# A different split of the first expert's weights, a shorter choice of that expert and larger, earlier clears in an attention and mixture-of-experts kernel

## What is computed

```python
h = x @ w_in                      # 512 x 2048
P = a[0] + a[1] * h + a[2] * h2 + a[3] * h3
Q = 1.0 + np.abs(b[0]) * np.abs(h) + np.abs(b[1]) * h2
g = P / (Q + 1e-06)
return (g @ w_out)                # 2048 x 512
```

## Time and profile before

| | us |
|---|---|
| three runs | 1037.04, 1037.2, 1035.95 (median 1037.04) |
| the profiled execution's own time | 1036.77 |
| its span in the profile | 1035.1 |
| PE busy in the span | 1003.8 (97%) |
| DVE, ACT, POOL busy | 647.5, 583.5, 410.9 |

### The profile page before, as it was taken

How to read it: one execution, slowest core, us unless ns; L and a number is a source line. 1 busy time by engine, 2 the same in 40 slices (tenths; PEclk the granted TensorE clock), 3 DMA queues, 4 the chain that set the end, 5 groups by cost and what they waited for, 6 DMA issues and landing times.

```text
span 1035.1 us, 19854 instructions
## 1 busy us (share of the span) xinstructions
PE 1003.8 (97%) x6222; PEld 819.4 (79%) x6223; DVE 647.5 (63%) x1207; ACT 583.5 (56%) x1255; POOL 410.9 (40%) x397
## 2 busy tenths in 40 slices
PE   8988999999999999999999999997999999999998
PEld 5777778888888888888888778786888888888886
DVE  5876788878867877887688679855223424325221
ACT  7877778766676667667666667624223324225221
POOL 3676444444543454455345357722111111112111
PEclk9999999999999999999999999998999999999999
DMA  8999614700920290064009942117311512411111
GB/s 301 357 403 348 256 41 135 232 1 11 314 84 0 100 307 0 10 234 163 0 18 373 366 149 72 41 42 294 123 41 48 190 42 84 159 41 40 31 48 37
DMA packets 58528, 143.26 MB, mean 138 GB/s; under 512 B 4967, under 2 KB 10727, under 8 KB 58480
## 3 DMA queue, kind: packets, MB, share of 16 engines
q1 hardware_dynamic: 51680, 121.07, 33.0%
q0 software_dynamic: 6800, 21.56, 6.2%
HBM read 71.08 MB, written 72.32 MB: 139 GB/s over the span
## 4 chain that ended last, share of the span: by engine, by line
PE 76%; issue 7%; SPq 5%; ACT 4%; DMA 3%; DVE 3%; POOL 1%; ACTq 0%; DVEq 0%; POOLq 0%
PE PS L511 20%; PE PS L670 19%; PE PS L542 14%; PE PS L551 13%; SPq L463 4%; PE PS L535 2%; ACT prob L819 2%; PE PS L613 2%; PE PS L690 2%; DMA x_raw<-w_exp 1%; PE PS L528 1%; DVE PS L1001 1%; DMA qk<-qk_all 1%; PE PS L583 1%; DMA e_raw<-w_exp 1%
## 5 line engine op out<-in xcount | busy, mean ns | idle before, releaser
L511 PE MATMUL PS<-xs,weights 128*128 (+1 forms) x1152 | 282.7, 394 | 0.0
L511 PEld LDWEIGHTS PS<-xs,weights 128*128 128x128 f32 x1152 | 212.6, 188 | 43.1
L670 PE MATMUL PS<-weights,g_hi 128*128 128x512 f32 x768 | 238.6, 392 | 7.6 <-POOL g_lo L1344 4.6
L1344 POOL TENSOR_TENSOR g_lo<-g_sb,g_hi 128x512 fp32r<-128x512 f32 x96 | 123.9, 1291 | 272.8 <-ACT g_hi L899 272.8
L670 PEld LDWEIGHTS PS<-weights,g_hi 128*128 128x128 f32 x768 | 142.8, 188 | 43.2 <-POOL g_lo L1344 9.1
L670 PE MATMUL PS<-weights,g_lo 128*128 128x512 f32 x384 | 149.6, 390 | 0.0
L542 PE MATMUL PS<-weights,xg_hi 128*128 (+1 forms) x448 | 143.3, 401 | 0.5 <-issue 0.2
L880 ACT ACTIVATE b_ln<-PS,cf 128x512 f32<-128x512 f32 x96 | 65.9, 686 | 132.8 <-PE PS L511 132.8
L551 PE MATMUL PS<-weights,h_hi 128*128 (+1 forms) x432 | 136.1, 396 | 0.1
L1347 POOL TENSOR_TENSOR den<-den,b_r 128x512 f32<-128x512 f32 x96 | 127.7, 1330 | 2.1 <-ACT b_r L907 2.1
L1099 DVE SCALAR_TENSOR_TENSOR den<-den,b_r 128x512 f32<-128x512 f32 x96 | 70.2, 731 | 50.9 <-POOL den L1347 50.9
(11 more groups left out here) (190 smaller groups left out, 1605.0 us busy)
## 6 DMA issues: line engine op xcount, KB each, us to landing
rows_by_expert<-pad_rows SPq DMA_DIRECT2D x40, 1028.0 KB, 15.1
e_raw<-w_exp SPq DMA_DIRECT2D x34, 512.0 KB, 6.7
qk<-qk_all SPq DMA_DIRECT2D x32, 480.0 KB, 6.6
vw<-v_all SPq DMA_DIRECT2D x32, 384.0 KB, 6.0
rows_by_expert<-pad_rows SPq DMA_DIRECT2D x8, 1285.0 KB, 18.2
w_raw<-w_mlp SPq DMA_DIRECT2D x16, 512.0 KB, 8.4
pad_rows<-rows_by_expert POOLq DMA_DIRECT2D x30, 257.0 KB
x_raw<-attention_out_t SPq DMA_DIRECT2D x10, 512.0 KB, 4.5
```

The source lines that it names most:

```text
L511: last = pe.matmul(PS[:, H_BANK + f % 2, :], w[:, wp], rhs, start=k == 0, stop=k == 3 * KT - 1)
L670: last = pe.matmul(PS[:, ACC_BANK + s, :], gp[:, f % 2, s * P:(s + 1) * P], w[:, wp], start=f == 0 and k == 0, stop=f == FT - 1 and k == 2)
L1344: pool.tensor_tensor(g_lo[:, q], g_sb[:], g_hi[:, q].bitcast(F32), ALU.subtract).then_inc(g_lo_done, 1)
```

## The change

```diff
-E_ACT = {4: 0, 6: 1, 8: 2, 9: 3, 10: 4, 12: 5, 13: 6, 14: 7}
-E_DVE = {6: 0, 10: 2, 12: 4, 14: 6}
-E_POOL = {7: 1, 11: 3, 13: 5, 15: 7}
+E_ACT = {5: 0, 7: 1, 9: 2, 11: 3, 12: 4, 13: 5, 14: 6, 15: 7}
+E_DVE = {6: (0,), 8: (1,), 10: (2,), 12: (3,), 14: (4, 5)}
+CLEARS = (0, 7, 14, 20, REGION)
...
-                for blk in ((b - 1,) if b < BLOCKS - 1 else (b - 1, b)):
-                    n = SUBS if blk < BLOCKS - 1 else SUBS + 1
+                if b < len(CLEARS):
+                    n = CLEARS[b] - CLEARS[b - 1]
                     for e in range(E):
-                        at = e * REGION + blk * SUBS
+                        at = e * REGION + CLEARS[b - 1]
...
                 if q >= STAGES:
-                    done = (q - STAGES) // 2 + 1
-                    sp.wait_ge(e0_pool if q % 2 else e0_dve, done)
+                    sp.wait_ge(e0_dve, q - STAGES + 1)
...
                     if st.m == 0:
                         pe.wait_ge(xg_lo_done, 1)
-                        pe.wait_ge(e0_dve, 3)
-                        pe.wait_ge(e0_pool, 3)
+                        pe.wait_ge(e0_dve, 6)
...
-            pe.wait_ge(e0_dve, WCH // 2)
-            pe.wait_ge(e0_pool, WCH // 2)
+            pe.wait_ge(e0_dve, WCH)
...
+            then = Chain(dve, first_chain)
             def choose_first():
-                then = Chain(dve, first_chain)
                 desc = cst[:, C_DESC:C_DESC + E]
                 dve.wait_ge(early_counts, 1)
                 then(dve.tensor_reduce(first_e[:, 1:2], PS[:, 6, 0:E], AX.X, ALU.max))
                 then(dve.scalar_tensor_tensor(early[:, 0], PS[:, 6, 0:E], first_e[:, 1:2], desc, ALU.is_equal, ALU.mult))
                 then(dve.tensor_reduce(first_e[:, 2:3], early[:, 0], AX.X, ALU.max))
-                then(dve.tensor_scalar(first_e[:, 0:1], first_e[:, 2:3], -1.0, float(E), ALU.mult, ALU.add))
-                then(dve.tensor_scalar(first_e[:, 3:4], first_e[:, 0:1], float(REGION), None, ALU.mult))
-                dve.tensor_scalar(sched[:, R_CNT, 4:5], first_e[:, 3:4], 1.0, None, ALU.add)
-                dve.tensor_copy(sched[:, R_CNT, 3:4], first_e[:, 3:4])
-                dve.tensor_copy(sched[:, R_CNT, 2:3], first_e[:, 0:1]).then_inc(first_ready, 1)
-                then(dve.tensor_scalar(first_e[:, 4:5], first_e[:, 3:4], -1.0, float(TCOLS), ALU.mult, ALU.add))
-                dve.wait_ge(first_ready, 1)
-                first = load_sched(dve, R_CNT, 2, 0, E - 1)
-                then(dve.tensor_copy(leap[:], cst[:, C_LEAP:C_LEAP + 2 * E][:, bass.ds(first, E)]))
-                then(dve.tensor_tensor(leap[:, E - 1:E], leap[:, E - 1:E], first_e[:, 4:5], ALU.add))
+                back = first_e[:, 2:3]
+                dve.tensor_scalar(sched[:, R_CNT, 3:4], back, -float(REGION), float(TCOLS), ALU.mult, ALU.add)
+                dve.tensor_scalar(sched[:, R_CNT, 4:5], back, -float(REGION), float(TCOLS + 1), ALU.mult, ALU.add)
+                dve.tensor_scalar(sched[:, R_CNT, 2:3], back, -1.0, float(E), ALU.mult, ALU.add).then_inc(first_ready, 1)
+            def rotate_first():
+                back = first_e[:, 2:3]
+                then.ran(dve.tensor_scalar(first_e[:, 0:1], back, -1.0, float(E), ALU.mult, ALU.add))
+                then.ran(dve.tensor_scalar(first_e[:, 3:4], back, -float(REGION), float(TCOLS), ALU.mult, ALU.add))
+                then(dve.tensor_scalar(early[:, 1], iota[:, 1:E + 1], back, -float(TCOLS), ALU.is_equal, ALU.mult))
+                then(dve.tensor_scalar(leap[:], early[:, 1], float(REGION), None, ALU.add))
+                then(dve.scalar_tensor_tensor(leap[:, E - 1:E], back, float(REGION), leap[:, E - 1:E], ALU.mult, ALU.add))
...
+                    if st.in_period(BLOCKS - 1) and st.m == 3:
+                        rotate_first()
                     if st.in_period(BLOCKS - 1) and st.m in E_DVE:
-                        split_early(E_DVE[st.m])
+                        for q in E_DVE[st.m]:
+                            split_early(q)
...
+            split_early(6)
             lower_x(1)
+            split_early(7)
             dve.wait_ge(w2_done, STEPS)
...
                     if r[0] == 0:
-                        pool.wait_ge(cleared, st.i * (16 * E))
+                        pool.wait_ge(cleared, 16 * E * (len(CLEARS) - 1) if st.in_period(BLOCKS - 1) else st.i * (16 * E))
...
-                        pool.wait_ge(cleared, 16 * E * BLOCKS)
+                        pool.wait_ge(cleared, 16 * E * (len(CLEARS) - 1))
...
-                if st.in_period(BLOCKS - 1) and st.m in E_POOL:
-                    split_early(E_POOL[st.m])
...
-F_AT = (4, 9)
-X_AT = (6, 7, 8)
+F_AT = (2, 9)
+X_AT = (4, 4, 5)
```

More of the change, by code:

```diff
@@ L327, in build @@
         last_read, early_counts = sem("last_read"), sem("early_counts")
-        e0_dve, e0_pool = sem("e0_dve"), sem("e0_pool")
+        e0_dve = sem("e0_dve")
         route_chain, sched_chain, sched_ready = sem("route_chain"), sem("sched_chain"), sem("sched_ready")
@@ L474, in _ @@
                 if q >= STAGES:
-                    done = (q - STAGES) // 2 + 1
-                    sp.wait_ge(e0_pool if q % 2 else e0_dve, done)
+                    sp.wait_ge(e0_dve, q - STAGES + 1)
                 sp.dma_start(early_buffer(q), w_exp[bass.ds(first, 1), c].rearrange("o p n -> (o p) n")).then_inc(eraw_in[c], 16)
-            sp.wait_ge(e0_dve, WCH // 2)
-            sp.wait_ge(e0_pool, WCH // 2)
+            sp.wait_ge(e0_dve, WCH)
             sp.wait_ge(h_ready, STEPS)
@@ L1305, in split_w @@
                 pool.tensor_tensor(wslice(c, 1, pool), raw, wslice(c, 0, pool).bitcast(F32), ALU.subtract).then_inc(w_lo_done, 1)
[L1307 to L1312, removed]
             def fetch(t, col):
```

## The result

The changed kernel took 1027.57 us (median of 6 runs, 1025.47 to 1028.75) against 1037.12 (6 runs, 1034.54 to 1038.62): ratio 0.9908, 95% interval 0.9891 to 0.9925. That is faster, as forecast, but 0.23 us under the lower end of the range. The same kernel measured again later gave 1028.10 against 1035.92, 0.9935 (0.9918 to 0.9951). All twelve runs of the changed kernel have a mean of 1028.1 and lie between 1025.5 and 1030.9; 82 runs of the kernel before, over all comparisons here, have a mean of 1036.8 and lie between 1033.0 and 1041.4. The gain is thus about 8 to 9 us, and even two sets of runs say it no better than that.

What follows compares the result with a forecast made beforehand. PE, busy 97% of the span, was taken as the bound. Of 8.67 us lost in the last block 1.14 would stay, a gain of 7.5 from 1036.77 to 1029.2; range 1027.8 to 1032.8.

Steps and rivals of the forecast that it cites:

- (a): Last block, step 2: PE waits 2.48 us for DVE's copies behind the long choice; shortening it gains 2.3.
- (c): Last block: three PE stalls, together 2.81 us, each following a POOL split that holds DVE back; removal gains about 4.5.
- (b): Last block: PE stalls 1.12 us as the expert's first weight chunk is issued behind clears; removal gains 1.3 to 1.5.
- The residues: Losses expected to stay in the last block: 0.44 in step 2, 0.5 in step 14, 0.2 at the last split.
- step 14: Last block, two DVE splits in one step beside POOL's product: a stall of 0.5 us, bounds 0 and 1.2.
- the last split: DVE's split behind the second tile's low part, end of the last block: costs 0.2 us, 1.2 without cover.
- 8.67: All the time in us that PE loses in the last block, stalls and restarts together, before the change.
- The signs: Expected in the later profile: L1099 at 0.69 throughout, L1347 at 2.26 or L1041 up to 2.5 five or six times.
- 1 (mutual waits add up): Rival: DVE's and POOL's waits accumulate, 0.8 us stalls in three or four of steps 7 to 14; 1031.5, chance 0.2.
- 2: Rival: the first tile or a chunk is late, PE stands in step 4 for 2 to 4 us; 1032, chance 0.07.
- 3: Rival: the large clears delay the next blocks through SP's list; 1080 at 150 GB/s, chance 0.04.
- 4: Rival: the choice isn't shorter, its 1.37 us register load appears elsewhere or the copies are held; 1031.4, chance 0.05.

Runs made afterwards that it cites:

- e1_after_again: The changed kernel measured once more with nothing altered: 1028.10 us, ratio 0.9935.
- e3_clears: The kernel before with only the clears in four rounds added: 1035.57 us, ratio 1.0001.
- g12_before_again: The kernel before measured once more with nothing altered: 1035.70 us, 0.9985 beside other runs of the identical kernel.
- e4_dve_alone: The kernel before with only the splits changed, all low parts on DVE in the new steps: 1031.99 us, ratio 0.9963.
- e5_choice_back: The changed kernel with the long choice of before and no rotate_first: 1031.55 us, ratio 0.9952.
- e2_choice: The kernel before with only the shorter choice and rotate_first added: 1036.99 us, ratio 1.0008.
- g11_before_warm: The kernel before with 14 short matmuls on zeros in PE's gap of step 2: 1038.33 us, ratio 0.9995.

## Why the forecast was right in its steps and wrong at its edge

- **Where the time was lost.** Right. 7.94 of 8.1 are in the stretch named; blocks 1 to 4 stay at 93.3. All three causes are real: undoing (a) or (c) brings back its own stalls, and stall (b) is gone with the clears alone.
- **(a) The choice.** Forecast 2.3; undoing it costs 2.0, the register load being 0.3 shorter with the new clears. In step 2 0.46 is left, forecast 0.44. The choice to copies, 0.85, was forecast to the hundredth.
- **(b) The clears.** Forecast 1.3 to 1.5. By difference it is 7.94 - 2.0 - 4.3 = 1.6. No gap is left at the fourth part of the output, and ACT takes the chunk at 601.96 without a marked wait. The fetch went out at 585.16 and no step waits for it.
- **(c) POOL's splits.** Forecast about 4.5; 4.2 and 4.3 from the two sides.
- **What the forecast left out: the order of the causes.** It treated them as a sum, which holds for undoing (a) or (c). Done alone they are worth -2.2, 0.15 and 3.6 in their traces, together 1.5 and not 7.9. Of this the lower clock took 1.6 from (a) and 1.1 from (b), which another execution might not have lost; with both given back it is some 4.2, still 3.7 short. Most of that is (a), whose 2.3 are waited again at (b)'s stall, and (c), with which the same stall is 0.6 larger. And the price of the early fetch without the spread clears, 13 us at its stall, was not seen: the prediction named PE's step 4 as the one that would wait, not the `g_lo` behind the fetch on POOL.
- **The residues were too large.** Forecast 0.44 + 0.5 + 0.2 = 1.14. Measured: 0.46 in step 2, at most 0.1 in step 14 (its lower bound was nothing), and for the last split at most 0.1: the copies start at 671.95, 0.09 behind ACT's at 671.86. The undisturbed block would be 113.98 - 8.67 = 105.31, and it is 106.04, so 0.7 of the 8.67 is left, 0.4 less than forecast. The block also began 0.12 earlier than in the trace before (565.91 for 566.03). With the rounding that puts the profiled execution, 1028.64, 0.6 under the forecast.
- **The signs.** L1345, the product that was L1347, took 2.25 to 2.28 five times and L1041 2.31 once, as foreseen (five or six times), and L1099 stayed at 0.69.
- **The step that failed: the lower end of the range, with the tail as a constant and 0.3 for the spread.** The end was 8.67 under one execution, less "0.3 for the spread of the runs". The stretch behind the last part of the output was called 355 "as before"; in the profiled executions it is from 350.8 to 355.5, in part with the granted clock. That both profiled executions, 355.09 and 355.05, lie at its long end is chance. The start of the last block moves as well, once by 4.2. The twelve runs of the changed kernel thus spread over 1025.5 to 1030.9, up to 2.7 us to either side of their mean, and medians of six can differ by one: the first set came out at 1027.57, the second at 1028.10. The mean of the twelve, 1028.1, lies inside the range, 1.1 under the forecast. Of that 0.6 is what the profiled execution shows too; the tail of `e1_after_again` is 1.3 shorter than 355.05, which would do for the rest, but where the unprofiled runs lost or won isn't known.
- **The rivals.** 1 (mutual waits add up) didn't occur: no stall in the steps 7 to 15. Single waits did, such as 2.28 for the product and 2.31 for the split in step 14, and the slack took them. 2 and 3 didn't occur. 4 neither: no register load moved to another place on the path.

## What to carry to other kernels

Stalls that follow one another in one block are not a sum. Ask of each what is late next if it goes: a moment that a DMA sets does not move with the engine, so a microsecond won in front of it is only waited longer. When a transfer is issued earlier, look at what stands behind its wait on the issuing engine, and not only at who uses its data. And before a range is stated, read how much one kernel's executions differ and where (here the granted clock behind short matmuls), instead of holding one execution's long tail for a constant.

## What the runs showed of the hardware

- A gap of PE of 2.2 to 2.5 us was followed by the lower clock in two executions (`e3_clears`, `g12_before_again`: pairs of 1.05 to 1.19, granted 0.88 in 576 to 590) and not in the profiled ones of before, `e4_dve_alone` and `e5_choice_back` (1.00). Where it was, step 2 took 1.1 and 1.5 us longer than in the trace of before. A stall of 4.04 in `e2_choice` was followed by it (a pair of 1.22), one of 3.16 in `g11_before_warm` wasn't (0.73).
- The time of a run goes with its mean granted clock: 66 runs of the kernel before beside the experiments lie on a slope of some 0.7 us for each 0.001 of clock (correlation -0.69).
- Small operations of DVE are held back beside POOL too. L1034 in `rotate_first`, 8 elements for each partition and one input, took 1.21 us where its neighbours take 0.15 to 0.38, while POOL was at its product; it lay beside other work and cost nothing here. From the timelines of DVE and of POOL, changed kernel:

```profile
589.63 1.21 DVE L1034 TENSOR_SCALAR leap<-early 128x8 f32<-128x8 f32 x1
```

```profile
589.53 1.28 POOL L1345 TENSOR_TENSOR den<-den,b_r 128x512 f32<-128x512 f32 x1
```

It ended at 590.84, 0.03 behind POOL's product. The kernel before has more such rows. Its routing's L1140, two inputs of 8 elements, takes 0.15 at 632.58 and 2.37 beside a POOL split:

```profile
644.71 2.37 DVE L1140 TENSOR_TENSOR posx<-posx,hot 128x8 f32<-128x8 f32 x1
```

```profile
644.66 2.40 POOL L1311 TENSOR_TENSOR weights<-e_raw,weights 128x1024 fp32r<-128x1024 f32 x1
```

They end at 647.08 and 647.06. L1135 there, one input like L1034's, took 1.02 at 631.57 and ended 0.02 behind POOL's product (631.28, 1.29). Not every small instruction is held: L1031 and L1032, of one element, took 0.15 and 0.14 at 589.09 and 589.15, while POOL was at `g_lo` (588.28, 1.29).
